# Moving the first instructions of two routings ahead of the ends of their blocks, and splitting the second gate's product into three bfloat16 parts

## The reference: attention, then two mixtures of experts

```python
x = attention(q, k, v)                    # banded: 96 local keys, 8 global keys; 4 x 8 heads, 768 x 64
# first mixture: top 1 expert, no capacity
do = x @ w_skip > 0                       # tokens that go through an expert at all
logits = x[do] @ w_gate; e = argmax(logits)
x[do] += softmax(logits)[e] * (relu(x[do] @ w1[e]) @ w2[e])
# second mixture: each token is given once, each expert takes N / E tokens, best logits first
logits2 = x @ w_gate2
assigned = greedy(order=argsort(-logits2.flatten()), capacity=384)
out[assigned == e] = relu(x[assigned == e] @ w1b[e]) @ w2b[e]
```

## Time and profile before

| | us |
|---|---|
| time of the kernel, median of 3 runs (808.31 to 808.92) | 808.35 |
| the profiled execution's own time | 809.03 |
| its span in the trace | 807.3 |
| TensorE busy in the span | 752.7 (93%) |
| VectorE busy | 536.9 (67%) |
| ScalarE busy | 453.4 (56%) |
| GpSimd busy | 165.3 (20%) |
| TensorE's mean granted clock, share of full speed | 0.975 |

### The profile page before, as it was taken

One profiled execution on the slowest core, in us unless ns is written; L12 is line 12 of the kernel. 1 busy time (PEld: TensorE's weight loads), 2 busy tenths in 40 slices (PEclk: granted clock), 3 DMA queues, 4 the chain that ended last, 5 costly groups with the idle time before them and its releaser, 6 DMA issues. The chain is left out here.

```text
span 807.3 us, 15740 instructions
## 1 busy us (share of the span) xinstructions
PE 752.7 (93%) x5588; PEld 676.4 (84%) x5590; DVE 536.9 (67%) x1463; ACT 453.4 (56%) x919; POOL 165.3 (20%) x184
## 2 busy tenths in 40 slices
PE   2899999999869999999999929999999999999997
PEld 2899999999738998899988816888888888888895
DVE  6877878778388768775566557666676767675420
ACT  3899999989425545465454304555545454636360
POOL 8100000000030322213221101141414142323221
PEclk9999999999979999999999957999999999999999
DMA  8999989986265457634663007868676777769861
GB/s 180 218 214 251 227 195 251 217 227 177 107 180 196 156 216 250 217 129 165 228 233 122 18 2 248 201 198 202 204 188 209 186 220 187 220 180 303 225 126 44
DMA packets 64106, 151.65 MB, mean 188 GB/s; under 512 B 12294, under 2 KB 15750, under 8 KB 64016
## 3 DMA queue, kind: packets, MB, share of 16 engines
q1 hardware_dynamic: 52512, 114.77, 48.6%
q0 software_dynamic: 11504, 35.72, 18.3%
HBM read 118.84 MB, written 16.67 MB: 168 GB/s over the span
## 5 line engine op out<-in xcount | busy, mean ns | idle before, releaser
L1817 PE MATMUL r_ph<-r_xh,r_w1h 128*128 128x384 f32 x256 | 90.7, 354 | 0.0
L1817 PE MATMUL r_ph<-r_xh,r_w1l 128*128 128x384 f32 x256 | 86.2, 337 | 0.0
L1817 PE MATMUL r_ph<-r_xl,r_w1h 128*128 128x384 f32 x256 | 85.8, 335 | 0.0
L592 ACT ACTIVATE pr<-pr,nmx 128x232 f32<-128x232 f32 (+1 forms) x192 | 79.9, 467 | 4.1 <-DVE nmx L685 2.6
L1098 PE MATMUL m_ph<-m_xh,m_w1h 128*128 128x224 f32 x288 | 81.0, 281 | 0.1
L1252 ACT ACTIVATE m_hh<-m_ph 128x224 fp32r<-128x224 f32 (+1 forms) x72 | 25.1, 349 | 98.0 <-PE m_ph L1098 94.1
L1098 PE MATMUL m_ph<-m_xh,m_w1l 128*128 128x224 f32 x288 | 79.1, 275 | 0.0
L1098 PE MATMUL m_ph<-m_xl,m_w1h 128*128 128x224 f32 x288 | 79.0, 274 | 0.0
L685 DVE CUSTOM_DVE_ANT_0 pr<-sc,bias 128x232 f32<-128x232 f32 (+1 forms) x192 | 65.1, 375 | 19.4 <-PE sc L466 16.4
L599 ACT ACTIVATE prt<-tp 128x384 f32<-128x384 f32 (+1 forms) x128 | 65.3, 535 | 20.4 <-PE tp L478 17.0
L1831 PE MATMUL r_py<-r_w2h,r_hh 128*128 128x512 f32 x192 | 76.1, 397 | 0.0
(11 more groups left out here) (298 smaller groups left out, 1960.7 us busy)
## 6 DMA issues: line engine op xcount, KB each, us to landing
r_w<-moe_w SPq DMA_DIRECT2D x64, 512.0 KB, 5.1
m_w<-moe_w SPq DMA_DIRECT2D x36, 512.0 KB, 5.6
row_buf<-moe_w SPq DMA_DIRECT2D x9, 2048.0 KB, 8.7
r_w2l<-r_w POOLq DMA_DIRECT2D x32, 512.0 KB, 4.9
k_raw<-kI SPq DMA_DIRECT2D x64, 208.0 KB, 7.2
q_raw<-qT SPq DMA_DIRECT2D x64, 192.0 KB, 8.2
vo<-vL SPq DMA_DIRECT2D x16, 384.0 KB
x_rows<-row_buf SPq DMA_DIRECT2D x4, 1536.0 KB, 6.6
```

Of the source, the lines that this page charges most:

```text
L592: nc.scalar.activation(pr[n % PRS][:, t, lo:CW], pr[n % PRS][:, t, lo:CW], ACT.Exp, bias=nmx[n % PRS][:, t:t + 1], scale=-1.0).then_inc(ex ...
L1817: last = nc.tensor.matmul(ph[m % 4][:, 0:CAP], w[:, c, m * P:(m + 1) * P], x[:, c, :], start=(c == 0 and a == 0), stop=(c == KC - 1 and a ...
```

## The change

It does four things.

1. The first seven VectorE instructions of `route` (up to `hot`) stand at the end of block one (`open_route`), behind the copy of the logits. TensorE's wait on `asked` is gone, since the block's end stands between. The tiles are allocated for the whole program.
2. The first VectorE instructions of block three (up to the first `candf`) stand at the end of block two (`open_search`). To allow it, the branches of VectorE on the number of overflow blocks are put in another order: the cases n < 1 and n > 1 are tested ahead of the overflow block's work, no longer behind it.
3. For blocks 0 to 6 the second gate's product uses three bfloat16 parts of the turned rows and three of `wg2`: all nine combinations, as 24 products of 24 columns (2 tiles, 4 chunks, 3 parts of the rows; the 3 parts of `wg2` stand side by side), instead of 8 float32 products of 8 columns. ScalarE makes parts 0 and 1, VectorE the remainders, and VectorE's last step sums the three groups of columns. The second tile is loaded with 128 columns instead of 96, the last 32 set to zero. Blocks 7 and E keep float32.
4. `z_part` has four steps, after m in `(1, 3, 4, 7)`; for block 7's rows, worked out in block E, after `(2, 3, 4, 5)`. Clearing `xg` moves from GpSimd to ScalarE, and `count_extra` gets four more instructions that split `wg2`.

```diff
+                def open_route(link):
+                    dve.wait_ge(filled, FILLS + 3)
+                    link(v.tensor_reduce(best1[:], logits[:, :, 0:E], AX.X, ALU.max))
...
+                    link(v.tensor_tensor(hot1[:], work1[:], live1[:].unsqueeze(1).broadcast_to(by_expert), ALU.mult))
...
+                    dve.wait_ge(read, B)
+                    open_route(link)
...
-            Z_AT, OVER_AT = (2, 3, 5), 3
+            Z_AT, Z_LAST, OVER_AT = (1, 3, 4, 7), (2, 3, 4, 5), 3
...
+            def in_parts(k):
+                return isinstance(k, int) and k < E - 1
...
-                for s in range(2):
-                    g.memset(xg[s][:], 0.0).then_inc(cleared, 1)
                 g.memset(never[:], NO_ROW).then_inc(cleared, 1)
-                pool.wait_ge(cleared, 3)
+                for part in y_parts:
+                    g.memset(part[:, :, WIDE1:], 0.0).then_inc(cleared, 1)
+                pool.wait_ge(cleared, 6)
...
+                    elif i == 3 and in_parts(k):
+                        pe.wait_ge(yt_kept, kept_before(k) + 6)
+                        pe.wait_ge(yt_low, kept_before(k) + 6)
+                        if k == 0:
+                            pe.wait_ge(cleared, 6)
+                        for t in tiles(k):
+                            for c in range(KC):
+                                for a in range(3):
+                                    last = nc.tensor.matmul(pt[0][:, BLK + t * 3 * E:BLK + (t + 1) * 3 * E], y_parts[a][:, c, t * P:t * P + P],
+                                                            wg2_parts[:, c].rearrange("p a e -> p (a e)"), start=(c == 0 and a == 0), stop=(c == KC - 1 and a == 2))
...
-                pe.wait_ge(asked, 1)
...
+                            dst = y_parts[0][:, c, 0:W] if in_parts(k) else yt[:, c, 0:W]
+                            nc.scalar.activation(dst, pt[c % 2][:, BLK:BLK + W], ACT.Copy).then_inc(yt_kept, 1)
+                    if i in (1, 2) and in_parts(k):
+                        two = slice(2 * i - 2, 2 * i)
+                        act.wait_ge(yt_low, kept_before(k) + 2 * i)
+                        nc.scalar.activation(y_parts[1][:, two, 0:WIDE1], yt[:, two, 0:WIDE1], ACT.Copy).then_inc(yt_kept, 1)
...
+                for s in range(2):
+                    nc.scalar.activation(xg[s][:].rearrange("p t d -> p (t d)"),
+                                         ones[:, 0:1].broadcast_to([P, TT1 * DM]), ACT.Copy, scale=0.0).then_inc(cleared, 1)
...
+                    if i < 2 and in_parts(k):
+                        for c in (2 * i, 2 * i + 1):
+                            dve.wait_ge(yt_kept, kept_before(k) + c + 1)
+                            v.tensor_tensor(yt[:, c, 0:WIDE1], pt[c % 2][:, BLK:BLK + WIDE1], y_parts[0][:, c, 0:WIDE1], ALU.subtract).then_inc(yt_low, 1)
+                    if i in (1, 2) and in_parts(k):
+                        two = slice(2 * i - 2, 2 * i)
+                        dve.wait_ge(yt_kept, kept_before(k) + 4 + i)
+                        v.tensor_tensor(y_parts[2][:, two, 0:WIDE1], yt[:, two, 0:WIDE1], y_parts[1][:, two, 0:WIDE1], ALU.subtract).then_inc(yt_low, 1)
...
+                            if in_parts(k):
+                                parts = pt[0][0:r, BLK + t * 3 * E:BLK + (t + 1) * 3 * E].rearrange("p (a e) -> p e a", e=E)
+                                last = v.tensor_reduce(zo[s][0:r, t, :], parts, AX.X, ALU.add)
...
+                def split_gate2():
+                    link(v.tensor_copy(wg2_parts[:, :, 0, :], wg2[:]))
+                    link(v.tensor_tensor(wg2_rest[:], wg2[:], wg2_parts[:, :, 0, :], ALU.subtract))
+                    link(v.tensor_copy(wg2_parts[:, :, 1, :], wg2_rest[:]))
+                    link(v.tensor_tensor(wg2_parts[:, :, 2, :], wg2_rest[:], wg2_parts[:, :, 1, :], ALU.subtract))
...
                 def count_extra():
+                    split_gate2()
...
+                with dve.If(n < 1):
+                    limits_of_all(Chain(dve, alone_chain))
+                with dve.If(n > 1):
+                    one_block(E, P)
...
                 with dve.If(n > 0):
-                    one_block(E, P)
                     with dve.If(n < 2):
+                        one_block(E, P)
...
                         put_z(alone)
...
+                        open_search(alone)
...
-                bests(logits2)
-                needs()
```

More of the change, by code:

```diff
@@ L808, in build @@
             by_expert = [P, E, NT]
[L809 to L810 removed]
+            hot, best, bestw, live = hot1, best1, bestw1, live1
             expd = tb("exp", shape)
             ranks, own, incl = (tb(x, by_expert) for x in ("ranks", "own", "incl"))
[L813 to L814 removed]
+            rank, high, gate, rest, away, total = (tb(x, [P, NT]) for x in ("rank", "high", "gate", "rest", "away", "total"))
+            low, col, gate1, gate2, gate3 = (tb(x, [P, NT], BF16) for x in ("low", "col", "gate1", "gate2", "gate3"))
             ranki, parti = tb("ranki", [P, NT], I32), tb("parti", [P, NT], I32)
@@ L1176, in _ @@
                 with pe.If(n < 1):
-                    for i in range(3):
+                    for i in range(4):
                         z_part(E - 1, 1, i)
@@ new lines, in limits_of_all, with more @@
+                def limits_of_all(alone):
+                    limit(alone)
+                    limit_all(alone)
+                    keep_limits(alone)
+                    open_search(alone)
+                def more(k):
+                    next_parts(k, 0, P)
+                    one_block(k, P)
+                    y_keep(k, 0)
+                    for i in range(4):
+                        z_part(k, 0, i)
+                with dve.If(n < 1):
+                    limits_of_all(Chain(dve, alone_chain))
@@ L1607, in build @@
             masked, tie, ranks = (tb(x, shape) for x in ("masked", "tie", "ranks"))
-            work, hot, gt, taken = (tb(x, shape, BF16) for x in ("work", "hot", "over", "taken"))
+            work, hot, best, bestm, bestw, need, needc, scr8, span, candf = (
+                work2, hot2, best2, bestm2, bestw2, need2, needc2, scr2, span2, candf2)
+            gt, taken = (tb(x, shape, BF16) for x in ("over", "taken"))
             firstb = firstb1
-            best, bestm, cmp1, rank1, high = (tb(x, [P, NT]) for x in ("best", "bestm", "cmp1", "rank1", "high"))
-            bestw, cmpb, ours, mem, upto, low = (tb(x, [P, NT], BF16) for x in ("bestw", "cmpb", "ours", "mem", "upto", "low"))
+            cmp1, rank1, high = (tb(x, [P, NT]) for x in ("cmp1", "rank1", "high"))
+            cmpb, ours, mem, upto, low = (tb(x, [P, NT], BF16) for x in ("cmpb", "ours", "mem", "upto", "low"))
             cmp_ = tb("cmp", [P, NT, RADIX], BF16)
```

126 lines of the change are left out of this document (71 added, 55 removed).

## The result

| | before | after | ratio, 95% interval |
|---|---|---|---|
| median of 4 runs, us | 808.62 (808.31 to 808.92) | 799.62 (798.62 to 800.69) | 0.9889 (0.9872 to 0.9906) |
| profiled execution, us | 809.03 | 798.62 | |
| its span, us | 807.3 | 796.9 | |

The kernel is 9.0 us faster (7.6 to 10.4 by the interval); the forecast was 7.2 and 801.1. The profiled execution after is the fastest of its four, so the two spans differ by more, 10.4 us.

The account below looks back on a forecast made before the run. TensorE was taken to bound the expert stretch, and the last engine to arrive the meetings at the block ends. Gains of 0.6 + 4.8 + 1.8 = 7.2 us took the median from 808.35 to 801.1, range 798.3 to 804.8.

Parts of the forecast that it names:

- What bounds the kernel: Expert stretch, 219.4 of 807.3 us: TensorE always has work, so work taken off it shortens the kernel one for one.
- The second gate's group: Blocks 0 to 6: 24 bfloat16 products replace a 1.50 us group, saving 0.74 per block; 4.8 us after a stall.
- the 0.1 for going back to float32r: Behind each new group: the next product takes 0.1 us more on return to float32, charged to the group's price.
- The chain of the parts: ScalarE copies and VectorE remainders ahead of each block's group: ready with 1.4 us or more to spare.
- The wait in block 1: Turning of block 0's second tile: longer `count_extra` makes TensorE wait 0.35 us.
- End of block one: Seven instructions moved ahead of the meeting gain only what they get cheaper by, `live` without GpSimd's clear: 0.6 us.
- End of block two: Search opened ahead of the meeting, TensorE's long branch no longer last: `cmpf` at 469.45 for 471.26, gain 1.8 us.
- (b): Rival, second gate's group: slow weight loads, 1.69 us like the strided group; gain of 0.7, 807.6 us; chance 0.05.
- (c): Rival, each block: fuller VectorE queue makes `hl` or parts 0.3 to 0.7 us late; 803.5 to 806.5 us; chance 0.09.
- (d): Rival, end of each block's steps: group waits for the parts' chain; at 1.6 us per block, 812.4 us; chance 0.04.
- (e): Rival, block ends: they give nothing, as moved work delays the meeting and VectorE's branch is long; 803.6 us; chance 0.08.
- (f): Rival, more gain: group at 0.55 without change-over, no stall, clock rising earlier behind block two; 797.5 to 799.3 us; chance 0.07.

Follow-up runs that it names:

- parts_only: Kernel before with the second gate's parts alone (points 3 and 4, clears of `xg` left on GpSimd): 801.45 us, ratio 0.9931.
- split4: Changed kernel with the four instructions splitting `wg2` moved from `count_extra` to behind step 4 of block 0: 799.71 us, ratio 0.9898.
- clears_act: Kernel before with only the two clears of `xg` moved from GpSimd to ScalarE: 807.53 us, ratio 0.9994.
- no_route: Changed kernel without `open_route`, its seven instructions behind the meeting again, clears of `xg` still on ScalarE: 799.47 us, ratio 0.9892.
- search_only: Kernel before with `open_search` and the new order of the branches alone: 805.94 us, ratio 0.9976.
- last_parts: Changed kernel with three bfloat16 parts for block 7's rows too, in block E behind steps 1, 3, 4 and 6: 800.42 us, ratio 0.9907.
- again: The changed kernel measured once more, unaltered, against the kernel before: 800.01 us, ratio 0.9892.
- strided: Changed kernel with the three row parts laid out so a product's 128 weight columns stand four elements apart: 807.51 us, ratio 0.9991.
- group5: Changed kernel with the group of 24 products behind step 5 instead of step 7: 816.06 us, ratio 1.0096.

## Why the prediction was right

- *What bounds the kernel.* Right. In the expert stretch the time went down by what TensorE's work did: 0.84 to 0.90 us from block to block in six blocks, and 0.41 in block 1.
- *The second gate's group*, 4.8 forecast, 5.58 in the trace (5.56 in parts_only, with a time to match): mis-sized by 0.8. The price of 0.66 for the 24 products was right (0.62). The term that was wrong is the 0.1 for going back to float32r: the old group had nearly the same change-over (behind it 0.186 us passed to the next product, 426.22 to 426.40, where 0.11 is the rule, so 0.08; behind the new one 0.32, 422.14 to 422.46, where the second product's first step takes 0.25 without a group ahead of it, 428.97 to 429.22 before, so 0.07), and it is no cost of the new one. The saving is 0.84 to 0.90 in a block, not 0.74. The chain of the parts was priced well: 1.4 us or more to spare was forecast, 1.41 measured. The wait in block 1 was forecast at 0.35 and was 0.40, for the reason given (split4).
- *End of block one*, 0.6 forecast, 0.58 in the trace. Both of its steps held: crossing the meeting gives nothing, the gain is GpSimd's clear leaving `live` alone. clears_act and no_route show it by the distances; in the times it is below what can be measured. Crossing even costs 0.2 in the trace. ScalarE's two clears, costed at nothing, took 2.0 us together, and what they delay, if anything, doesn't stand out of the scatter: from the count to h0 are 15.6 to 16.2 us with them, 15.7 to 15.8 without.
- *End of block two*, 1.8 forecast, 2.25 in the trace, 1.9 in the time of search_only: mis-sized. From the last opened instruction to `cmpf` I had some 0.95; it takes 0.5. The gain belongs in part to how long TensorE's branch happens to be: beside the parts alone (4.75) opening the search gains 1.1, beside the kernel before 2.25. In these profiles the two parts share this gain; summing the distances of parts measured alone counts 1.1 twice.
- *What is not the change.* The profiles differ by 10.4 us, the terms come to 8.4, and the medians to 9.0. The copy of the logits, ahead of which no instruction changed, stands between 219.2 and 220.4 in the 14 profiles; the two latest (search_only, no_route) are the two in which TensorE's clock also fell for 3.4 us at 28 us. `cmpf` to the end takes 334.7 to 336.6. And y(E) to the logits takes 10.9 to 12.1 us by when TensorE's clock falls in it. In the kernel before:

```profile
461.58:462.58 1.00, 0.65 (x5) 0.65 (x5) 0.61 (x3) 0.30 (x2) 0.44 (x1) 0.88 0.03 8
462.58:463.58 1.00, 1.00 (x6) 0.97 (x6) 0.08 (x1) 0.00 (x0) 0.00 (x0) 0.50 0.38 144
```

and in the changed one:

```profile
456.85:457.85 1.00, 0.43 (x2) 0.14 (x2) 0.52 (x3) 0.00 (x0) 0.00 (x0) 1.00 0.00 0
457.85:458.85 1.00, 0.00 (x0) 0.00 (x0) 0.90 (x3) 0.00 (x0) 0.00 (x0) 0.51 0.00 0
```

Before, the clock falls to 0.50 at 462.34, with the second gate's products still to do; after only at 457.87, behind the complete logits: the 0.91 us. The 14 profiles bear this out (last_parts aside, whose load was late): the fall 8.4 us behind y(E) goes with 12.09, 8.8 with 11.81, 9.2 with 11.41, 9.4 to 9.6 with 11.31 to 11.32, 10.2 with 11.03, and 10.4 or more with 10.89 to 10.91. In again, the same program, it is 11.31 instead of 10.90; so it varies from execution to execution, and the width of 1 us for the clock was right. Of the 1.5 us by which the median lies below the forecast, 1.2 are the terms (8.4 for 7.2); the rest is within the scatter.
- *The rivals.* (b), a group at 1.69, would not have come even with strides like that of strided (0.80), whose time came near (b)'s for another reason; (c) did not come, since `h_low` and the parts were never waited for; (d) is real and 1.4 us away (group5), and dearer than I priced it; (e) is contradicted by search_only; of (f) the missing change-over came, and a low stretch of the clock of 23.9 us for 30.7, but it was 27.3 in again.

## What to carry to other kernels

Moving instructions ahead of a meeting pays only on an engine that is not the last to arrive there. Ask who is last, and what the moved instructions were slow for: here the gain at one end was a neighbour's clear that had moved, and at the other a long branch of another engine that stopped being the last. When work is shifted from the bounding engine to others with a chain across them, measure the spare time at the consumer and keep to it: putting the group two steps sooner cost more than the whole change gave. Price a change-over on both sides of the edit before charging it to the new one.

## What was not expected of the hardware

- A bfloat16 product of 24 columns with its weight load costs 25.7 ns from start to start at 128 contiguous weight columns, 33 ns when they lie four elements apart, 45 ns at 96 columns, and 70 ns in block 0's group, 24 elements apart with 48 columns to stream. A single load is listed with 96, 118, 125 and 173 ns; the loads overlap.
- Writing bfloat16 four elements apart doubles ScalarE's and VectorE's time (354 to 742 ns, 587 to 1271, 618 to 1187).
- One VectorE instruction (TENSOR_SCALAR on 128x24 elements) took 0.93 us beside GpSimd's clear and ended with it, and 0.18 beside ScalarE's clear of the same tile; a reduction and a comparison of two tensors beside the same clears were not slowed.
- Waits of TensorE of 1.93, 1.48 and 1.47 us between busy stretches were followed by 3.4 us at half the granted clock; waits of 1.52, 1.28, 1.26 and 1.23 us in the four other blocks were not (group5).
